# The first load in four transfers, and the rows of the first stores dealt anew

## What is computed

```
kv  = einsum('bhsd,bhse->bhde', k, v)
out = einsum('bhsd,bhde->bhse', q, kv)
out = out / sqrt(mean(out * out, axis=-1) + 1e-6) * g_norm
x   = out as (4608 tokens, 512)
logits = x @ phi                           # (4608, 32 slots)
d = softmax of logits over the tokens      # dispatch
slot_input = d.T @ x                       # (32, 512)
slot_out[e] = relu(slot_input[e] @ w1[e]) @ w2[e]
c = softmax of logits over the slots       # combine
result = c @ slot_out                      # (4608, 512)
```

## Time and profile before

| | us |
|---|---|
| median of 3 runs (171.64 to 171.88) | 171.77 |
| the profiled execution, its own time | 171.68 |
| its span, first to last instruction | 170.4 |
| TensorE busy in the span | 147.3 |
| ScalarE busy | 88.9 |
| VectorE busy | 87.3 |
| GpSimd busy | 59.9 |

### The profile page before, as it was taken

The page is one execution under the profiler, slowest core; times in us unless marked ns, Lnnn a source line. Parts: engine busy times, 40 slices in busy tenths (PEclk is TensorE's granted clock), DMA queues, the critical chain, the costliest instruction groups (busy, mean ns, idle before and its releaser), DMA issues.

```text
span 170.4 us, 4230 instructions
## 1 busy us (share of the span) xinstructions
PE 147.3 (86%) x1832; PEld 104.0 (61%) x1832; DVE 87.3 (51%) x185; ACT 88.9 (52%) x230; POOL 59.9 (35%) x73
## 2 busy tenths in 40 slices
PE   7887899899899899999988999899989789989200
PEld 3466779799679787887885673455645343454000
DVE  1122159683676564847266999427884137219300
ACT  3127588787966878869498870113221045218300
POOL 7000707777556477382646589000000004000000
PEclk9999999999999999999999999999999999999855
DMA  5999999999999999999999899999899999999996
GB/s 184 426 431 424 431 425 427 493 419 465 441 413 407 458 428 419 485 400 424 473 409 485 350 458 442 400 421 473 343 423 431 442 444 400 419 428 418 427 436 300
DMA packets 3844, 71.65 MB, mean 421 GB/s; under 512 B 778, under 2 KB 778, under 8 KB 913
## 3 DMA queue, kind: packets, MB, share of 16 engines
q1 hardware_dynamic: 3425, 71.20, 97.8%
q0 software_dynamic: 400, 0.18, 0.4%
HBM read 61.94 MB, written 9.44 MB: 419 GB/s over the span
## 4 chain that ended last, share of the span: by engine, by line
PE 54%; DMA 24%; ACT 11%; DVE 3%; issue 1%; SPq 1%
PE psum L92 54%; DMA arena<-in_w_dram 16%; DMA arena<-in_kv_dram 8%; ACT arena L92 3%; ACT bd L92 3%; ACT sq L92 2%; ACT part L92 1%; SPq L92 1%; DVE ms L92 1%; ACT r L92 1%; ACT d L92 1%; DVE logits L92 1%; DVE d L92 0%; DVE part L92 0%; DVE arena L92 0%
## 5 line engine op out<-in xcount | busy, mean ns | idle before, releaser
L92 PE MATMUL psum<-bd,arena 128*128 128x192 f32 (+1 forms) x320 | 54.7, 335 | 2.8 <-ACT bd L92 1.6
L92 PEld LDWEIGHTS psum<-bd,arena 128*128 128x128 f32 (+1 forms) x320 | 45.3, 179 | 8.3 <-ACT bd L92 2.8
L92 PE MATMUL psum<-arena 128*64 128x64 f32 (+2 forms) x896 | 37.6, 270 | 3.3 <-DMA arena<-in_w_dram 1.2
L92 PEld LDWEIGHTS psum<-arena 128*64 128x64 f32 (+2 forms) x896 | 27.3, 129 | 15.0 <-issue 4.1
L92 DVE TENSOR_REDUCE ms<-sq 128x16 f32<-128x1024 f32 (+1 forms) x19 | 22.1, 1163 | 26.3 <-ACT sq L92 25.9
L92 POOL TENSOR_TENSOR arena<-arena,r 128x512 f32<-128x512 f32 x34 | 34.8, 1044 | 0.0
L92 POOL TENSOR_TENSOR part<-part,r 128x512 f32<-128x512 f32 x17 | 17.9, 1050 | 47.4 <-DVE r L92 47.4
L92 ACT COPY arena<-psum 128x512 f32<-128x512 f32 (+2 forms) x48 | 30.7, 649 | 6.0 <-PE psum L92 5.9
L92 ACT ACTIVATE sq<-psum 128x512 f32<-128x512 f32 x36 | 21.5, 597 | 10.6 <-PE psum L92 10.3
L92 ACT COPY part<-psum 128x256 f32<-128x256 f32 (+1 forms) x38 | 13.6, 359 | 10.0 <-DVE part L92 8.8
L92 DVE TENSOR_REDUCE logits<-part 128x64 f32<-128x512 f32 (+1 forms) x18 | 17.8, 991 | 0.1
(11 more groups left out here) (75 smaller groups left out, 108.6 us busy)
## 6 DMA issues: line engine op xcount, KB each, us to landing
arena<-in_w_dram SPq DMA_DIRECT2D x2, 8064.0 KB, 30.4
arena<-in_t_dram SPq DMA_DIRECT2D x1, 6912.0 KB, 37.6
arena<-in_w_dram SPq DMA_DIRECT2D x1, 6400.0 KB, 23.2
arena<-in_w_dram SPq DMA_DIRECT2D x3, 2048.0 KB, 19.6
arena<-in_kv_dram SPq DMA_DIRECT2D x2, 2304.0 KB, 23.4
arena<-in_kv_dram SPq DMA_DIRECT2D x1, 4608.0 KB, 42.7
arena<-in_w_dram SPq DMA_DIRECT2D x1, 4096.0 KB, 24.1
arena<-in_kv_dram SPq DMA_DIRECT2D x1, 3584.0 KB, 32.3
```

What stands on the lines that cost most here:

```text
L92: self.inst, self.token = method(*args, **kwargs), None
```

## The change

There are two edits, and the rest only makes room for them (`kv_landed` now holds lists of semaphores).

The first load becomes four transfers, all issued one behind the other on SP: rows 0, 8, 16 and so on (16 rows), rows 4, 12, 20 and so on (16 rows), rows 2, 6, 10 and so on (32 rows), and the odd rows (64). Their readers wait for all four.

In `FIRST` the transfer to five engines has 25 rows in place of 30, so one row less for each of engines 0 to 4. The first transfer on GpSimd's queue has 24 rows on two engines in place of 20, and its second has 5 rows in two chunks (ten pieces) in place of 9 rows in one chunk, on one engine. The small pieces for engine 0 keep their sizes and start at other rows.

```
 FIRST = (
-    ("sync", 1, 4, 30, 5, 1, 0, 1), ("sync", 121, 4, 2, 3, 3, 0, 1), ("sync", 117, 4, 3, 2, 2, 1, 2),
-    ("gpsimd", 1, 4, 20, 2, 1, 1, 2), ("gpsimd", 81, 4, 9, 2, 2, 1, 2),
+    ("sync", 1, 4, 25, 5, 1, 0, 1), ("sync", 101, 4, 2, 3, 3, 0, 1), ("sync", 97, 4, 3, 2, 2, 1, 2),
+    ("gpsimd", 1, 4, 24, 2, 1, 1, 2), ("gpsimd", 109, 4, 5, 2, 2, 0, 2),
     ("sync", 3, 4, 32, 1, 1, 0, 2), ("sync", 0, 2, 64, 1, 1, 0, 3), ("sync", 1, 2, 64, 1, 1, 2, 3),
 )
...
-    kv_landed[0, 0] = dma(sp, arena[:, : HEAD + 2304], first_in)
+    n = HEAD + 2304
+    kv_landed[0, 0] = [dma(sp, arena[p::step, :n], first_in[p::step]) for p, step in ((0, 8), (4, 8), (2, 4), (1, 2))]
...
-            after=[kv_landed[0, 0], gphi_zero],
+            after=[*kv_landed[0, 0], gphi_zero],
...
-                        after=[slots_done.get(self.b - 1), kv_landed[self.b, g]],
+                        after=[slots_done.get(self.b - 1), *kv_landed[self.b, g]],
```

More of the change, by code:

```diff
@@ L203, in soft_moe_linear_attention @@
     kv_landed, q_landed = {}, {}
-    kv_landed[0, 0] = dma(sp, arena[:, : HEAD + 2304], first_in)
-    kv_landed[0, 1] = load_row(KV_AT[0] + 9, kv_in[0, :, 2304:])
+    n = HEAD + 2304
+    kv_landed[0, 0] = [dma(sp, arena[p::step, :n], first_in[p::step]) for p, step in ((0, 8), (4, 8), (2, 4), (1, 2))]
+    kv_landed[0, 1] = [load_row(KV_AT[0] + 9, kv_in[0, :, 2304:])]
     q_landed[0, 0] = load_row(Q_AT[0], q0_in[:, :2048])
-    kv_landed[1, 0] = load_row(KV_AT[1], kv_in[1, :, :2304])
-    kv_landed[1, 1] = load_row(KV_AT[1] + 9, kv_in[1, :, 2304:])
+    kv_landed[1, 0] = [load_row(KV_AT[1], kv_in[1, :, :2304])]
+    kv_landed[1, 1] = [load_row(KV_AT[1] + 9, kv_in[1, :, 2304:])]
     q_landed[0, 1] = load_row(Q_AT[0] + 8, q0_in[:, 2048:])
-    kv_landed[2, 0] = kv_landed[2, 1] = load_row(KV_AT[2], kv_in[2])
+    kv_landed[2, 0] = kv_landed[2, 1] = [load_row(KV_AT[2], kv_in[2])]
     q_landed[1, 0] = load_row(Q_AT[1], q1_in)
@@ L748, in soft_moe_linear_attention @@
     bd_set[0] = [[halves_set[0][1], halves_set[1][0]], [halves_set[1][1]]]
-    kv_landed[3, 0] = kv_landed[3, 1] = load_row(KV_AT[3], kv_in[3], after=[kv.read])
-    q_landed[1, 1] = kv_landed[4, 0] = kv_landed[4, 1] = load_row(Q_AT[1] + 8, kv4_in)
-    q_landed[2, 0] = q_landed[2, 1] = kv_landed[5, 0] = kv_landed[5, 1] = load_row(KV_AT[5], kv5_in)
+    kv_landed[3, 0] = kv_landed[3, 1] = [load_row(KV_AT[3], kv_in[3], after=[kv.read])]
+    q_landed[1, 1] = load_row(Q_AT[1] + 8, kv4_in)
+    kv_landed[4, 0] = kv_landed[4, 1] = [q_landed[1, 1]]
+    q_landed[2, 0] = q_landed[2, 1] = load_row(KV_AT[5], kv5_in)
+    kv_landed[5, 0] = kv_landed[5, 1] = [q_landed[2, 0]]
     def load_t3():
@@ L755, in load_t3 @@
         for key in ((6, 0), (6, 1), (7, 0), (7, 1)):
-            kv_landed[key] = landed
+            kv_landed[key] = [landed]
         q_landed[3, 0] = q_landed[3, 1] = landed
```

## The result

The changed kernel takes 172.94 us (172.66 to 173.49) where the kernel before takes 171.78 beside it (171.64 to 171.94), 6 runs each: a ratio of 1.0072, with a 95% interval of 1.0055 to 1.0089. A second measurement, in a later session, gave 1.0095 (1.0069 to 1.0121). The span of the profiled run is 171.4 us, 1.0 more than before.

What follows compares the result with a forecast made beforehand. The prediction took the DMA engines as the bound: profiled 171.68 us, less 0.44 for the first load, plus 0 for the stores, gives 171.24; plus 0.09 for the median, 171.33, stated as 171.3. Its own range was 170.95 to 171.65.

Steps and rivals of the forecast that it cites:

- What bounds the kernel: Whole run: DMA engines, full from 10.25 to 140.25 us, set the end; an earlier start passes through, computing doesn't replace it.
- The first load: Start of the run: four transfers lose 0.20 us in place of 0.64, a gain of 0.44; bounds 0 to -0.64.
- the pace: SP's issues at the start: the four transfers were taken to issue 0.46 us apart, as the first four issues before.
- The third rival: First load's first two transfers: 16 stepped rows reach eight of sixteen SBUF ports, full DMA shares at half GB/s; chance 0.09.
- its mild form: The smaller slowdown allowed to the third rival at the first load, reaching to 172.1 us.
- The second rival: First load: SP's issue pace becomes the bound, slower beyond 0.68 us apart, 172.6 us at 0.96; chance 0.07.
- The first rival: Start: slow for a reason shape does not touch, 157 GB/s again up to 2.75 us; 171.6 to 172.0; chance 0.34.
- The rule against the change: First load: skill advises 128 partitions per transfer; about 2 us each, three times 2 us more, run near 178.
- The stores: Last store's new deal over DMA engines: taken as 0, with bounds -0.23 and +0.46 us.
- The range: Whole run: forecast's own 170.95 to 171.65 us, said to come from its bounds.

Runs made afterwards that it cites:

- the split alone: First load in the change's four stepped transfers, stores dealt as in the kernel before: 174.0 us, 1.0134 against that kernel; repeated in another session, 173.26 us, 1.0084.
- the quarters: Kernel before, with its first load in four transfers of all 128 rows, each a quarter of the columns: 172.55 us, 1.0042.
- the packed pieces: Kernel before, with its first load in the change's four stepped sets of SBUF rows, each reading neighbouring HBM rows: 173.63 us, 1.0109.
- two columns: Kernel before, with its first load in two transfers of all 128 rows, each half of the columns: 171.81 us, 1.0001.
- blocks: Kernel before, with its first load in four transfers of neighbouring rows (0 to 15, 16 to 31, 32 to 63, 64 to 127): 174.82 us, 1.0173.
- blocks of 64 rows: Kernel before, with its first load in two transfers of neighbouring rows, 0 to 63 and 64 to 127: 174.33 us, 1.0142.
- the deal alone: Kernel before, with only the stores dealt anew (new `FIRST`) and the first load whole: 171.97 us, 1.0002.

## Why the prediction was wrong

**What bounds the kernel** was right. In the changed kernel the loss of the start, 0.94 us, is nearly all of the span's 1.0; 10.25 to 140.25 stayed at 431 to 433 GB/s in all versions, and computing hid none of it. Three versions lost more than their start: the split alone (1.14 at the start, 1.9 in the span), the quarters (1.67 and 2.9) and the packed pieces (1.22 and 2.0). In all three a lone row of the last store starts half a microsecond or more behind the others. In the quarters it is this one:

```profile
171.25:171.75 0.50, 0.00 (x0) 0.00 (x0) 0.00 (x0) 0.00 (x0) 0.00 (x0) 0.50 0.00 0
171.75:172.00 0.25, 0.00 (x0) 0.00 (x0) 0.00 (x0) 0.00 (x0) 0.00 (x0) 0.50 0.23 98
```

Over 0.25 us, 98 GB/s are one row of 24576 bytes. So one DMA engine was left behind there. Which one, and why, is open.

**The first load** is the step that failed: -0.44 was forecast, +0.93 came. The bounds themselves (0 to -0.64) were wrong, since no reason excluded a loss. Two of its assumptions fell. First, the pace: 0.46 apart was taken from whole loads, and pieces came 0.65 apart, with first bytes later as well. The trace of the changed kernel has no row started from 1.75 to 2.00, where eight started before:

```profile
1.75:2.00 0.25, 0.25 (x2) 0.12 (x1) 0.16 (x1) 0.25 (x1) 0.03 (x1) 1.00 0.00 0
2.00:2.25 0.25, 0.25 (x2) 0.04 (x1) 0.00 (x0) 0.02 (x1) 0.25 (x2) 1.00 1.30 353
```

By the prediction's own sum that gives 2 x (0.65 - 0.36) = 0.58 idle between pieces and at least 0.25 at the start: 0.83 lost in place of 0.64, or 0.2 slower; by the DMA shares it was some 0.3. Second, and larger, a row was priced at 0.36 us whichever rows go together. That was good for whole loads only. By the shares, rows that took longer are some 0.6 of the 0.94 lost, and the second load in pieces, with its queue full, lost 0.44 to 0.49 in this way. What makes stepped rows take longer stays open: it is not HBM's side (the packed pieces lost no less), and either the rows that a piece writes in SBUF or a cost of each further transfer would do. The latter, as three more semaphore writes, the prediction put at nothing; two columns agree with that for one further transfer, and no run makes three without also changing which rows go together or how long they are.

That small unstepped pieces start at once was right (470 GB/s in the first quarter with blocks), and so worthless, because they are the ones that write slowest.

**The third rival** came nearest, with a chance of 0.09 and a price of +0.29 for its mild form. Its sign, full DMA shares at half the GB/s, is there from 2.75 to 4.25 (0.98, 216), though not from 1.75 on. Its reason, pairs of DMA engines at one port, no run shows, and blocks, without any step, were the slowest. The argument against it was read from stores, which read SBUF; loads in pieces, which write it, came out otherwise. The Trainium skill, SBUF — State Buffer, section Door 1: The DMA port swizzle, says that rows 0 to 63 reach only half of the ports and that a transfer's rows set its rate. For writing, 219 GB/s in blocks of 64 rows, half of 432, agree with it. The sixteen-row blocks agree in direction. That the quarters lose is no statement of that section; which DMA engine writes which row may matter, and no view shows that. **The second rival**'s pace of 0.68 was nearly met (0.65), and it put the loss at nothing there, since it left out the later first bytes. **The first rival**'s row, 157 GB/s up to 2.75, is there, but the rows are not the same: none starts before 2.00, and by the shares the first nine last 0.58 us each, where the first eight lasted 1.09 before.

**The rule against the change** was right in its direction and too large in its price: three further transfers cost about 1 us, not 6. The Trainium skill, DMA: Bandwidth & Descriptors, section Rules for kernel authors, gives another reason for its advice than the prediction has: two transfers to halves of the partitions share the same engines. No view here names engines.

**The stores** at 0 were right: 1.0002 for the deal alone.

**The range** of the forecast does not come from its bounds: -0.64 - 0.23 and 0 + 0.46 give 170.90 to 172.23, not 170.95 to 171.65. With the rivals it ended at 172.1, from the mild form of one slower one, and 172.94 lies beyond. By the prediction's prices two of them together, with the later first bytes, give 0.58 + 0.25 + 0.73 in place of 0.64, that is 0.92 slower or 172.7. They were weighed one by one, and both held in part.

## What to carry to other kernels

Loads of all 128 whole rows ran at full rate, and every subset of rows that was tried lost time. A piece with fewer or shorter rows has to be shown to run at full rate, in the same direction, before a row of it is priced so. A low rate alone does not say that engines were idle: read the DMA share beside the GB/s. To put a transfer's cost between bounds, ask for a reason on each side: "no worse than now" is a claim like any other. When a slow start is split into more transfers, the issue of the pieces has to be read from pieces.

## What the runs showed of the hardware

Writing 64 neighbouring rows of SBUF went at 219 GB/s with all DMA engines busy, however HBM was read (218), and all 128 rows in one transfer at 432. Issues on SP took 0.39 us for 128 rows and 0.56 to 0.65 for stepped pieces of 16 to 64. Stepped pieces of 16 and 32 rows, queued behind 3 us of work, went at 307 GB/s with all engines busy. A first load in quarters of its columns carried 242 GB/s in its first microsecond where the whole rows carried 157, but its rows of 2448 bytes took about 0.14 us each, not 0.09, behind it.
